# Issuing two transfers of a rotated-query tile from ScalarE instead of SP, in a one-core attention and mixer kernel

## The reference, cut to what matters

```
q_rot, k_rot = rotate(q), rotate(k)                 # (4, 8, 576, 64)
scores = scale * (q_rot @ k_rot^T)
attn = exp(scores - max) / (sum + 1e-9)
x = (attn @ v) laid out as (4, 576, 512)
u = x + (relu(x^T @ w_tok1) @ w_tok2)^T
out = u + relu(u @ w_ch1) @ w_ch2
```

## Time and profile before

| what | us |
|---|---|
| three runs: median (lowest to highest) | 640.83 (640.73 to 640.95) |
| span of the profiled execution | 639.1 |
| PE busy in the span | 621.5 |
| DVE busy | 509.4 |
| ACT busy | 464.2 |
| POOL busy | 341.0 |

### The profile page before, as it was taken

One profiled execution on the slowest core, in us unless ns is written; L12 is line 12 of the kernel. 1 busy time (PEld: TensorE's weight loads), 2 busy tenths in 40 slices (PEclk: granted clock), 3 DMA queues, 4 the chain that ended last, 5 costly groups with the idle time before them and its releaser, 6 DMA issues.

```text
span 639.1 us, 13808 instructions
## 1 busy us (share of the span) xinstructions
PE 621.5 (97%) x4724; PEld 604.7 (95%) x4724; DVE 509.4 (80%) x877; ACT 464.2 (73%) x1016; POOL 341.0 (53%) x316
## 2 busy tenths in 40 slices
PE   3899999999999999999999999999999999999997
PEld 3799999999999999999999999999999999999997
DVE  6899999999999999987385985569935499553895
ACT  3889999988889899986383664776556765567753
POOL 3999999998888887560900002860017800068200
PEclk9999999999999999999999999999999999999999
DMA  4767766767668774406001332000320002100002
GB/s 133 168 159 197 212 151 179 187 173 183 174 176 211 203 189 114 122 20 216 19 1 44 155 84 75 1 2 2 84 74 0 0 0 80 43 33 1 1 3 74
DMA packets 61898, 63.01 MB, mean 99 GB/s; under 512 B 18896, under 2 KB 46160, under 8 KB 61840
## 3 DMA queue, kind: packets, MB, share of 16 engines
q1 hardware_dynamic: 61392, 62.15, 35.7%
q10 hardware_dynamic: 448, 0.10, 0.1%
HBM read 31.46 MB, written 9.44 MB: 64 GB/s over the span
## 4 chain that ended last, share of the span: by engine, by line
PE 95%; SPq 1%; DVE 1%; DMA 1%; ACT 0%; issue 0%; ACTq 0%; DVEq 0%
PE slot L615 12%; PE rest L648 12%; PE rest L625 9%; PE slot L1344 8%; PE slot L1346 8%; PE slot L1345 8%; PE rest L1344 6%; PE rest L1346 6%; PE rest L1345 6%; PE rest L376 3%; PE rest L576 3%; PE rest L635 2%; PE slot L1376 2%; PE rest L1376 2%; PE rest L224 1%; PE rest L221 1%
## 5 line engine op out<-in xcount | busy, mean ns | idle before, releaser
L1335 POOL TENSOR_TENSOR w_ch_part<-w_ch_sums,w_ch_part 128x512 fp32r<-128x512 f32 x21 | 31.0, 1474 | 173.3 <-ACT w_ch_part L1588 173.3
L984 DVE TENSOR_REDUCE neg_max<-slot 128x1 f32<-128x576 f32 x142 | 106.7, 752 | 6.6 <-PE slot L615 2.2
L1652 ACT ACTIVATE pieces<-h 128x288 fp32r<-128x288 f32 x168 | 73.8, 444 | 49.8 <-PE slot L1346 25.3
L992 DVE TENSOR_TENSOR pt_lo<-rest,pt_hi 128x512 fp32r<-128x512 f32 x144 | 96.0, 677 | 1.9 <-ACT pt_hi L845 1.3
L648 PE MATMUL rest<-pt_hi,v 128*128 128x256 f32 (+1 forms) x320 | 89.3, 303 | 0.0
L845 ACT ACTIVATE pt_hi<-rest 128x512 fp32r<-128x512 f32 x144 | 84.1, 595 | 5.2 <-PE rest L625 4.3
L1743 DVE TENSOR_TENSOR pieces<-h,pieces 128x288 fp32r<-128x288 f32 x168 | 74.6, 454 | 9.4 <-ACT pieces L1652 8.9
L648 PE MATMUL rest<-pt_lo,v 128*128 128x256 f32 (+1 forms) x256 | 69.7, 295 | 0.0
L615 PE MATMUL slot<-key,q_hi 128*128 128x288 f32 x252 | 63.5, 333 | 2.2 <-ACT prob_a L838 1.0
L838 ACT ACTIVATE prob_a<-slot,neg_max 128x576 f32<-128x576 f32 x78 | 58.0, 743 | 10.1 <-DVE neg_max L984 10.0
L648 PEld LDWEIGHTS rest<-pt_hi,v 128*128 128x128 f32 x320 | 60.3, 188 | 0.1
(11 more groups left out here) (263 smaller groups left out, 2107.3 us busy)
## 6 DMA issues: line engine op xcount, KB each, us to landing
key<-t_hi_k SPq DMA_DIRECT2D x31, 144.0 KB, 2.3
key<-t_lo_k SPq DMA_DIRECT2D x31, 144.0 KB, 2.4
raw_qk<-in_q_dram SPq DMA_DIRECT2D x16, 256.0 KB, 2.8
raw_v<-in_v_dram SPq DMA_DIRECT2D x16, 256.0 KB, 3.3
x_scratch<-x_pair SPq DMA_DIRECT2D x16, 256.0 KB, 2.1
stage_or_x<-x_scratch SPq DMA_DIRECT2D x16, 256.0 KB, 4.3
q_hi<-t_hi_q SPq DMA_DIRECT2D x31, 128.0 KB, 2.4
q_cross<-t_hi_q SPq DMA_DIRECT2D x31, 128.0 KB, 2.4
```

The costliest lines, as they stand in the source:

```text
L984: dve.tensor_reduce(neg_max[p % 2][:, i:i + 1], slot[g if 2 <= g < 4 else g % 2][:, :, 0:HALF], AX.XY, ALU.max, negate=True).then_inc(maxe ...
L992: dve.tensor_tensor(pt_lo[:, :, cols], rest[:, bank, :].rearrange("p (j n) -> p j n", j=G), f32(pt_hi[:, 0:G, cols]), ALU.subtract).then_i ...
L1652: act.activation(pieces[:, ring(m), 0, :], source[WEIGHTS[n]][:, ft, :], ACT.Copy).then_inc(piece_hi, 1)
```

## The change

The two transfers of the rounded q for head A of pair 1 leave SP's order. ACT issues them, after it has rounded that q and before `exponent(0, 7)`, behind a wait for its own rounding and for four score tiles. SP still issues the three other transfers, and the semaphore still collects five.

```diff
@@ -422,9 +422,10 @@
                 return
             i = p % 2
             mine, other = halves(a)
-            sp.wait_ge(t_hi_done["q"], p + 1)
-            sp.dma_start(f32(q_hi[a][mine, :]), f32(t_hi["q"][i][mine, 0:MAIN])).then_inc(tiles_in[a], 16)
-            sp.dma_start(f32(q_cross[a][other, :]), f32(t_hi["q"][i][mine, 0:MAIN])).then_inc(tiles_in[a], 16)
+            if (a, p) != (0, 1):
+                sp.wait_ge(t_hi_done["q"], p + 1)
+                sp.dma_start(f32(q_hi[a][mine, :]), f32(t_hi["q"][i][mine, 0:MAIN])).then_inc(tiles_in[a], 16)
+                sp.dma_start(f32(q_cross[a][other, :]), f32(t_hi["q"][i][mine, 0:MAIN])).then_inc(tiles_in[a], 16)
             sp.wait_ge(t_lo_done["q"], p + 1)
             sp.dma_start(f32(q_cross[a][mine, :]), f32(t_lo["q"][i][mine, 0:MAIN])).then_inc(tiles_in[a], 16)
 
@@ -891,6 +892,10 @@
         t_part_hi("k", 1, 0)
         exponent(0, 6)
         t_part_hi("q", 1, 2)
+        act.wait_ge(scores, G)
+        act.wait_ge(t_hi_done["q"], 2)
+        act.dma_start(f32(q_hi[0][top, :]), f32(t_hi["q"][1][top, 0:MAIN])).then_inc(tiles_in[0], 16)
+        act.dma_start(f32(q_cross[0][low, :]), f32(t_hi["q"][1][top, 0:MAIN])).then_inc(tiles_in[0], 16)
         exponent(0, 7)
         turned_hi(0, 0, 1)
         tails_hi(0, 0, 0)
```

## The result

The changed kernel took 642.02 us (median of 21 runs, 641.49 to 642.92), the kernel before 641.08 in the runs beside it (21 runs, 640.73 to 641.89). The ratio is 1.0015, with a 95% interval of 1.0008 to 1.0021: 0.94 us slower, inside 0.2%, where 0.86 had been forecast. The interval stands for 0.5 to 1.3 us, so that the times alone can't tell 0.86 from 0.6 or 1.2; the traces can.

The account below looks back on a forecast made before the run. PE bounds the kernel, solid matmuls from score(1, 2) at 28.83 us. Shift = 1.24 + 0.19 - 0.20 - 0.37 = +0.86, so 640.83 + 0.86 = 641.7 us; own range 641.5 to 641.9, 8 in 10 640.4 to 642.3.

Parts of the forecast that it names:

- PE's block behind `score(1, 2)` passes a shift on: From 28.83 us PE runs a solid block of matmuls; moving that start moves the end by as much, forecast +0.86 us.
- the wait ahead of 272 us: Later idle place of PE; the forecast is wrong if it shrinks by what was lost at score(1, 2).
- P, the price of the pair: Time the two issues hold ACT before exponent(0, 7): taken as 1.24 us, with 1.10 and 1.40 for the range.
- the reading for an idle queue: Pair's price if its first issue goes into an idle queue, as on SP at 13.39: 0.46 + 0.04 + 0.60 = 1.10 us.
- DVE's slack of 0.20 and 0.37: Lateness DVE absorbs: 0.20 us at the first remainder, turned_lo(0, 0), and 0.37 us at maximum(1, 0).
- SP's side: SP issues q's remainder 0.65 us earlier, landing at 25.63 after the same 2.37; at most 0.37 us gained.
- ACT not held: Rival: an issue costs ACT next to nothing before exponent(0, 7), SP's 0.37 us is gained, 640.5 us; 12%.
- One issue's length: Rival: ACT is held by about one issue, 0.6 us, shift +0.2, 641.1 us; 12%.
- The falling clock: Rival: PE's longer pauses before 29.7 us lower its clock, costing 1.7 us on top of 0.86, 643.4 us; 7%.
- The slow queue: Rival: ACT's transfers land over 4.1 us after issue and hold score(1, 0), 642 to 643 us; 3%.

Follow-up runs that it names:

- e_pay: Kernel before, SP's five transfers unchanged, plus two same-size issues on ACT into an unread spare tile at the change's place; +1.30 us against the kernel before.
- e_later_small: Changed kernel with ACT's two issues moved after turned_hi(0, 0), each carrying 64 of 512 columns; -0.24 us against the kernel before.
- e_none: Changed kernel with the two transfers of the rounded q left out and semaphore counts lowered; -0.02 us against the kernel before.
- e_order: Kernel before, ACT untouched, all five transfers on SP, which issues the load of q of pair 2 after them; -0.12 us against the kernel before.
- r_order: Repeat of e_order, the load of q of pair 2 issued later on SP; +0.21 us against the kernel before.
- e_one: Changed kernel, but ACT issues only q_hi at the same place and SP issues q_cross and the remainder; +0.55 us against the kernel before.
- e_three: Changed kernel plus a third issue on ACT behind its two, into a spare tile; +1.83 us against the kernel before.
- e_later: Changed kernel with ACT's same two issues placed after turned_hi(0, 0), not before exponent(0, 7); +0.05 us against the kernel before.

## Why the prediction was right

- **PE's block behind `score(1, 2)` passes a shift on.** Held. M grew by 0.80 and 0.82, the times by 0.94 and 0.87; for `e_pay` 1.27 and 1.30. The other sign asked for, the wait ahead of 272 us, shrank by nothing (the first row is before, the second the changed kernel):

```profile
273.26 0.50 PE L615 MATMUL slot<-t_hi_k,t_hi_q 128*128 128x288 f32 x2 [0.53 <-ACT prob_a L838]
```

```profile
274.40 0.51 PE L616 MATMUL slot<-t_hi_k,t_hi_q 128*128 128x288 f32 x2 [0.53 <-ACT prob_a L839]
```

For gains the times can't tell: -0.40 in M gave -0.02, -0.24, -0.12 and +0.21, each with some 0.6 either way. In the traces `e_later_small` kept its gain (610.06 us from `score(1, 2)` to the end, against 610.27), `e_none` lost it to one late transfer, and `e_order` and `r_order` lost most of it ahead of head B's first score tile. That the change met +0.86 within 0.1 is the traces' finding; the time of 0.94 could have been 0.5 or 1.3.

- **P, the price of the pair.** The right mechanism, sized a little high: taken as 1.24, it was 0.50 + 0.03 + 0.62 = 1.15, closer to 1.10, the reading for an idle queue that was kept for the range. With the waits around it the exponential came 1.38 late relative to the rounding (24.15 - 22.17 against 22.26 - 21.66), against 1.43 forecast. The 50 ns that the Trainium skill gives for a dispatch ("DMA: Bandwidth & Descriptors", section "Anatomy of one DMA — SWDGE (gpsimd) path") are not what an issue on ACT's queue costs here, 0.50 and 0.62 us.
- **DVE's slack of 0.20 and 0.37.** Held: `turned_lo(0, 0)` 1.18 late (25.50 - 22.17 against 23.81 - 21.66), `maximum(1, 0)` 0.81 late (28.47 - 22.17 against 27.15 - 21.66). `e_one` and `e_three` put the slope on either side, `e_none` the floor.
- **SP's side.** Here a step failed, hidden by the longer path. "With the same 2.37 us it lands at 25.63", 0.65 earlier: the issue was indeed earlier, by 0.67 relative to the rounding (23.75 - 22.17 against 23.91 - 21.66), but the landing took 2.8 and 3.1. Relative to the rounding it landed at 4.38 and 4.69, against 4.62 before. What SP's relief was worth was 0.2 us or nothing. It was luck that this didn't count: DVE was the later of the two at that place, and in `e_pay`, where the landing took 3.6, it was not. The Trainium skill, "DMA: Bandwidth & Descriptors", section "Issuing engines are not separate DMA queues", says that transfers started by different engines run on the same 16 DMA engines and interleave. The traces agree as far as the bytes go (2.8 to 3.1 beside full-size transfers of ACT, 2.4 beside small ones); I had quoted that section and not drawn it into the sum.
- **The rivals.** ACT not held: false at the place of the change, half true elsewhere (`e_later`). One issue's length: false. The falling clock: not in the changed kernel, but real in the version with a third issue. The slow queue: ACT's own transfers landed in 2.3 to 2.7 us.

## What to carry to other kernels

Before moving an issue to another engine, look at what that engine hands on next and how much slack the receiver has: here 1.15 us of issues bought at most 0.2 us of landing, and of the 1.38 us by which they made the exponential late DVE's slack took only 0.57. If it has to be moved, put it behind the instructions that others wait for, so that its wait is already met and handed-over work covers it; the same two issues, two instructions later in the order, went out at the same times and cost nothing (and gained nothing). And an earlier issue is only an earlier landing if the bytes in front of it are not the same bytes moved to another queue.

## What the runs showed that I had not expected

- An issue on ACT ran beside an activation already handed over: 22.75 to 23.25 beside 22.56 to 23.30 in `e_later`.
- Landing of a 128 KB transfer inside SBUF: for SP's remainder at this place 2.2 to 2.4 us with SP's queue alone, 2.8 to 3.1 beside ACT's full-size transfers, 3.6 with two more transfers, 2.4 beside ACT's of 16 KB.
- Matmuls of 288 columns went back from some 290 to 442 ns after PE had paused for 2.0 us in two of two executions, with a granted clock of 0.50; at the start of the program the same 442 ns stand beside 1.00.
- The slow stretch at the start ended at 15.1 and at 17.7 us in two executions of the same kernel; the rounding of q came 9.46 us after the first score tile in the one and 9.15 in the other.
- The same operation on DVE, `w_ch_lo`, took 3.25 us in eleven traces and 3.70 and 3.74 in two, which put some 0.45 us on those two executions.
